# Linear attention and two MLPs on one core: where the second network's weights are split, and the order at the seams

## The reference

```python
# attention, 8 batches x 8 heads x 576 tokens x 64
q_s = exp(q - max(q, axis=-1)); q_s = q_s / (sum(q_s, axis=-1) + 1e-09)
k_s = exp(k - max(k, axis=2));  k_s = k_s / (sum(k_s, axis=2) + 1e-09)
x = q_s @ (k_s^T @ v)                      # -> 4608 tokens x 512
# first network: 512 -> 2048 -> 512
h = x @ w_in
g = np.maximum(h, 0.0) + alpha * np.minimum(h, 0.0)
y = g @ w_out
# second network: 512 -> 1024 -> 512
h = y @ w_in2
solu = h * softmax(h)
ln = (solu - mean(solu)) / np.sqrt(var(solu) + 1e-06) * g_ln
out = ln @ w_out2
```

## Time and profile before

| | us |
|---|---|
| median of 3 runs | 1254.08 (1253.91 to 1256.19) |
| the profiled execution | 1256.36 |
| its span, first to last instruction | 1254.5 |
| TensorE busy | 1221.4 (97%) |
| VectorE busy | 817.5 (65%) |
| ScalarE busy | 507.8 (40%) |
| GpSimd busy | 201.4 (16%) |
| mean granted TensorE clock | 0.988 of full |

### The profile page before, as it was taken

The page is one execution under the profiler, slowest core; times in us unless marked ns, Lnnn a source line. Parts: engine busy times, 40 slices in busy tenths (PEclk is TensorE's granted clock), DMA queues, the critical chain, the costliest instruction groups (busy, mean ns, idle before and its releaser), DMA issues.

```text
span 1254.5 us, 16472 instructions
## 1 busy us (share of the span) xinstructions
PE 1221.4 (97%) x6129; PEld 1010.7 (81%) x6129; DVE 817.5 (65%) x1054; ACT 507.8 (40%) x716; POOL 201.4 (16%) x175
## 2 busy tenths in 40 slices
PE   8889999999999999999999999997999999999998
PEld 7768888888888787888888888985888888888887
DVE  7757577585673556878767697666755655556553
ACT  4433434334343334444344444434543443444432
POOL 5533323133231000000000000011211111111110
PEclk8999999999999999999999999998999999999999
DMA  9686675766744544261452715442544444444432
GB/s 240 210 232 202 176 233 156 222 220 176 227 133 163 204 168 154 104 228 68 152 183 68 228 41 184 153 133 69 176 143 151 144 142 140 150 140 145 143 126 76
DMA packets 199725, 200.74 MB, mean 160 GB/s; under 512 B 62936, under 2 KB 147440, under 8 KB 199536
## 3 DMA queue, kind: packets, MB, share of 16 engines
q1 hardware_dynamic: 199616, 199.91, 50.8%
q10 hardware_dynamic: 48, 0.01, 0.0%
HBM read 116.45 MB, written 83.42 MB: 159 GB/s over the span
## 4 chain that ended last, share of the span: by engine, by line
PE 91%; DVE 4%; DMA 1%; SPq 1%; ACT 1%; issue 1%; POOL 0%; ACTq 0%; DVEq 0%
PE ps_y L1536 10%; PE ps_y L1537 10%; PE ps_y L1538 10%; PE ps_y L1671 5%; PE ps_y L1673 5%; PE ps_y L1672 5%; PE ps_y L1622 5%; PE ps_y L1626 5%; PE ps_y L1624 5%; PE ps_h L1646 3%; PE ps_m L1622 3%; PE ps_h L1647 3%; PE ps_h L1651 3%; PE ps_m L1626 3%; PE ps_m L1624 3%; PE ps_m L1647 2%
## 5 line engine op out<-in xcount | busy, mean ns | idle before, releaser
L1536 PE MATMUL ps_y<-X,W 128*128 128x512 f32 x576 | 228.4, 397 | 3.0 <-DVE gst L1163 3.0
L1537 PE MATMUL ps_y<-X,W 128*128 128x512 f32 x576 | 226.0, 392 | 0.0
L1538 PE MATMUL ps_y<-X,W 128*128 128x512 f32 x576 | 225.9, 392 | 0.0
L1163 DVE SCALAR_TENSOR_TENSOR gst<-gst,nslope,ps_y 128x512 f32<-128x512 f32 x144 | 104.8, 731 | 153.9 <-ACT gst L822 153.8
L822 ACT ACTIVATE gst<-ps_y 128x512 f32<-128x512 f32 x144 | 85.7, 597 | 267.8 <-PE ps_y L1538 250.0
L740 POOL TENSOR_TENSOR x2lb<-x2r,x2hb 128x512 fp32r<-128x512 f32 x36 | 47.1, 1309 | 689.8 <-ACT x2hb L957 689.8
L1536 PEld LDWEIGHTS ps_y<-X,W 128*128 128x128 f32 x576 | 109.1, 189 | 27.1 <-DVE gst L1163 3.4
L1538 PEld LDWEIGHTS ps_y<-X,W 128*128 128x128 f32 x576 | 109.1, 189 | 23.2
L1537 PEld LDWEIGHTS ps_y<-X,W 128*128 128x128 f32 x576 | 109.1, 189 | 22.2
L1622 PE MATMUL ps_y<-rh,WOc 128*128 128x512 f32 (+1 forms) x320 | 117.8, 368 | 1.4 <-DVE rl L1290 1.4
L1624 PE MATMUL ps_y<-rl,WOc 128*128 128x512 f32 (+1 forms) x320 | 117.7, 368 | 0.0
(11 more groups left out here) (176 smaller groups left out, 2303.0 us busy)
## 6 DMA issues: line engine op xcount, KB each, us to landing
g_scratch<-gst SPq DMA_DIRECT2D x144, 256.0 KB, 2.3
RX<-g_scratch SPq DMA_DIRECT2D x36, 512.0 KB, 3.6
z_scratch<-zb SPq DMA_DIRECT2D x35, 512.0 KB, 2.6
zt<-z_scratch SPq DMA_DIRECT2D x140, 128.0 KB, 2.8
RY<-g_scratch SPq DMA_DIRECT2D x18, 512.0 KB, 4.4
RZ<-g_scratch SPq DMA_DIRECT2D x18, 512.0 KB, 5.1
x2r<-y_scratch SPq DMA_DIRECT2D x36, 256.0 KB, 3.1
KK<-k_dram SPq DMA_DIRECT2D x16, 512.0 KB, 6.3
```

Source lines behind the costliest of these rows:

```text
L1163: nc.vector.scalar_tensor_tensor(gst[:, n % 3, :], gst[:, n % 3, :], nslope[:, f:f + 1], ps_y[:, f % 4, :], ALU.mult, ALU.add).then_inc(g_ ...
L1536: nc.tensor.matmul(o, W1[:, f, 0, a, :], x[:, 0, a, :], start=(a == 0), stop=False)
L1537: nc.tensor.matmul(o, W1[:, f, 0, a, :], x[:, 1, a, :], start=False, stop=False)
L1538: mm = nc.tensor.matmul(o, W1[:, f, 1, a, :], x[:, 0, a, :], start=False, stop=(a == KT - 1))
```

## The change

- **Weights of the second network.** `w2_split`, `w2_high`, `w2_low` and their loads are gone. Instead 16 pieces of 128 x 512 (eight of w_in2, eight of w_out2) are loaded into `wst`, split into `whl` (high on ScalarE, low on VectorE) and stored, high and low, to a DRAM scratch `ws_scratch`, three pieces in each of chunks 1 to 5 and one in chunk 6. When the w_out pieces that lie on their place have been used, GpSimd issues six DMAs (two of 2 MB, four of 1 MB) that load `W2` and `WO2`, ready split.
- **Third tile of the second network.** Product 1 of tile 2 goes to the first two banks of `ps_y` (`h_bank`), and waits for `c12_ok` in place of `solu_ok`. For tiles 0 to 3 the orders of ScalarE and VectorE are written out.
- **First chunk.** `k_transpose` from f = 1 to 3, `k_broadcast` 3 to 5, `k_columns` 2 to 3, `k_sub` 4 to 6, third `q_sum` 6 to 7, `k_exp` 7 to 8, `kv_product` and what follows it one step later; the low halves of the first two q tiles for chunk 1 on VectorE instead of GpSimd.
- **Seams.** In chunk 7 the `xrg` split moves from f = 3 to 6 and 7, the w_out pieces from f = 6, 9, 12, 15 to 8, 11, 14 and 1 of chunk 8; in chunk 8 from 5, 9, 13 to 4, 8, 12. The first two units of phase 2 are split ahead of the PReLUs of f = 14 and 15 instead of both ahead of f = 15.

```diff
+        def h_bank(m, r):
+            if isinstance(m, int) and m == 0 and r == 2:
+                return ps_y[:, 0:2, :]
+            return (ps_m, ps_h)[r % 2][:, :, :]
...
+        WS_LOAD, WS_SPLIT = (1, 6, 10), (4, 10, 13)
+        def ws_piece(c, i):
+            n = 3 * (c - 1) + i
+            return n if c > 0 and n < WS else None
...
+            def load_ws(n):
+                if n < 2:
+                    sp.wait_ge(w_lo, NF)
+                else:
+                    sp.wait_ge(ws_lo, n - 1)
...
+                sp.dma_start(wst[:, n % 2, :], src).then_inc(ws_in[n % 2], 16)
+            def store_ws(n):
+                sp.wait_ge(ws_lo, n + 1)
+                sp.dma_start(ws_dram[n].rearrange("s p n -> p s n"), whl[:, :, :].bitcast(F32)).then_inc(ws_st, 16)
...
+                    if f in WS_LOAD and ws_piece(c, WS_LOAD.index(f)) is not None:
+                        load_ws(ws_piece(c, WS_LOAD.index(f)))
+                    if f - 1 in WS_SPLIT and ws_piece(c, WS_SPLIT.index(f - 1)) is not None:
+                        store_ws(ws_piece(c, WS_SPLIT.index(f - 1)))
...
+            pool.wait_ge(ws_st, 16 * WS)
+            for n in range(2):
+                pool.wait_ge(b_used, ends(LAST_U, n))
+                pool.dma_start(W2[:, n, :, :].rearrange("p a (h n) -> p (a h) n", h=2),
+                               ws_dram[0:2 * KT, n, :, :].rearrange("m p n -> p m n")).then_inc(w2_in, 16)
+            half = NF2 // 2
+            for n in range(2):
+                pool.wait_ge(b_used, ends(LAST_U, 2 + n))
+                for i in range(2):
+                    pool.dma_start(WO2[:, n * half:(n + 1) * half, i, :],
+                                   ws_dram[2 * KT + n * half:2 * KT + (n + 1) * half, i, :, :]
+                                   .rearrange("m p n -> p m n")).then_inc(wo2_in, 16)
...
+            def ws_high(n):
+                act.wait_ge(ws_in[n % 2], 16 * (n // 2 + 1))
+                if n > 0:
+                    act.wait_ge(ws_st, 16 * n)
+                if n < 2 * KT:
+                    nc.scalar.activation(whl[:, 0, :], wst[:, n % 2, :], ACT.Copy).then_inc(ws_hi, 1)
...
             for f in range(NF):
-                if f == NF - 1:
-                    for t in UNITS[:EARLY]:
-                        b_high(t)
+                if f >= NF - EARLY:
+                    b_high(UNITS[f - (NF - EARLY)])
                 negative(LAST, f)
-                if f in (5, 9, 13):
-                    wo_high(4 + (5, 9, 13).index(f))
+                if f == 1:
+                    wo_high(3)
+                if f in (4, 8, 12):
+                    wo_high(4 + (4, 8, 12).index(f))
...
                     if t.u == LAST_U:
-                        if t.k in (2, 3):
-                            w2_split(2 * (t.k - 2))
-                            w2_split(2 * (t.k - 2) + 1)
                         if t.k in (4, 5):
...
+            def ws_low(n):
+                dve.wait_ge(ws_hi, n + 1)
+                if n < 2 * KT:
+                    nc.vector.tensor_tensor(whl[:, 1, :], wst[:, n % 2, :], whl[:, 0, :].bitcast(F32),
+                                            ALU.subtract).then_inc(ws_lo, 1)
...
                 if first and r == 0:
-                    pe.wait_ge(w2_lo, KT)
+                    pe.wait_ge(w2_in, 32)
                     pe.wait_ge(c11_ok, PAIRS + 1)
...
+                if first and r == 2:
+                    pe.wait_ge(c12_ok, 2 * (PAIRS + 1))
+                if not (first and r < 3):
                     pe.wait_ge(solu_ok, i - 1)
```

More of the change, by code:

```diff
@@ L74, in linear_attention_two_mlps @@
         X = (X0, X1)
-        (qTh, qTl, kvh, kvl, KK, Q, QN, V, _, kb, qz, wst, kmax, kmt, kvf, qR, xr, arows, kx, ky, kw, kwt, km, ks, kr,
+        (qTh, qTl, kvh, kvl, KK, Q, QN, V, _, kb, qz, wst, whl, kmax, kmt, kvf, qR, xr, arows, kx, ky, kw, kwt, km, ks, kr,
          qm, qs, qe, qr) = place(
@@ L201, in linear_attention_two_mlps @@
         y22_st = sem("y22_st")
-        w2v_in = sem("w2v_in")
-        w2a_in = sem("w2a_in")
-        w2_hi = sem("w2_hi")
-        w2_lo = sem("w2_lo")
+        ws_in = [sem(f"ws_in{i}") for i in range(2)]
+        ws_hi = sem("ws_hi")
+        ws_lo = sem("ws_lo")
+        ws_st = sem("ws_st")
+        w2_in = sem("w2_in")
+        wo2_in = sem("wo2_in")
         x2_in = [sem(f"x2_in{i}") for i in range(4)]
@@ L727, in _ @@
                 w_low(f)
-            for j in range(KT):
+            for j in range(2, KT):
                 q_low(1, j)
@@ L1008, in out_copy, with tiles @@
                 nc.scalar.activation(ost[:, r % 2, :], ps_y[:, 2 + r % 2, :], ACT.Copy).then_inc(o_ok, 1)
-            def tiles(m, first=False, second=False, last=False):
+            def tiles(m, second=False, last=False):
                 for r in range(4):
                     if r >= 2:
-                        zt_high(m, r - 2, first=first)
-                    elif not first:
+                        zt_high(m, r - 2)
+                    else:
                         zt_high(m - 1, r + 2)
@@ L1018, in tiles @@
                         x2_high(m + (r + 2) // 4, (r + 2) % 4)
-                    if first and r < 2:
-                        for f in range(4 * r, 4 * r + 4):
-                            w2_high(f)
                     square_tile(m, r)
                     if r == 3:
-                        out_copy(m, 0, first=first, last=last)
-                    elif not first:
+                        out_copy(m, 0, last=last)
+                    else:
                         out_copy(m - 1, r + 1, first=(second and r == 0))
-            tiles(0, first=True)
+            exp_tile(0, 0)
+            x2_high(0, 2)
+            square_tile(0, 0)
+            exp_tile(0, 1)
+            x2_high(0, 3)
+            square_tile(0, 1)
+            exp_tile(0, 2)
+            x2_high(1, 0)
+            zt_high(0, 0, first=True)
+            square_tile(0, 2)
+            zt_high(0, 1, first=True)
+            exp_tile(0, 3)
+            x2_high(1, 1)
+            square_tile(0, 3)
+            out_copy(0, 0, first=True)
             tiles(1, second=True)
@@ L1228, in _ @@
                         if f == 6:
+                            k_sub(b)
+                        if f == 7:
                             q_sum(b, 2)
@@ L1270, in _ @@
                 prelu(B - 1, f)
-                if f == 3:
-                    for j in range(KT):
+                if f in (6, 7):
+                    for j in range(2 * (f - 6), 2 * (f - 5)):
                         dve.wait_ge(xh_ok, 4 * B + j + 1)
```

182 lines of the change are left out of this document (92 added, 90 removed).

## The result

The changed kernel takes 1251.49 us (median of 10 runs, 1249.44 to 1253.61); the kernel before, run beside it, 1256.26 us (10 runs, 1253.83 to 1258.75). The ratio is 0.9962, with a 95% interval of 0.9952 to 0.9972: faster by 0.38%, 4.8 us. The forecast was 7.9 us less, so the sign was right, and two fifths of the forecast gain are missing. In absolute time 1251.49 us is 5.3 more than the forecast 1246.2: 3.1 us are the missing gain, and 2.2 come from the kernel before, whose median over three runs was 1254.08.

A forecast was written before the change was run, and what follows sets the result against it. The prediction took TensorE's waits, and the half-rate clock after long ones, as the bound (TensorE is 91% of the chain). Terms 0 + 0 + 0 + 1.0 - 0.3 - 8.6 = -7.9 us took 1254.08 to 1246.2 us, range 1240 to 1252.

The forecast's parts named there:

- First chunk: Chunk 0: kmax wait goes, but TensorE waits elsewhere, the x product's wait growing 3.2 to 4.6 us; net 0, bounds -2.5, +2.
- The weights' waits of 2 us near 51 us: First chunk: TensorE, now early, waits some 2 us for the eighth weight tile, which came by DMA only at 51.8 us.
- Splits in chunks 1 to 6: Splitting the second network's weights there costs 0, using 3.0 of 3.5 us of slack; bounds 0 and +5 us.
- the nearest deadline: Chunks 1 to 6: the third tile's x product, 3.5 us of slack between its qTl and its start.
- Chunk 7: The 3.0 us gst wait, from g stores behind 5 MB of loads, stays and the clock falls as before; 0.
- Seam: Start of w_out phase: 1.8 us wait goes, unit 2 waits 3.0 for RY; +1.0 us, or 0.65 gain without low clock.
- Last unit group: 801 to 844 us: one 1.35 us wait goes, but GpSimd's loads slow the RX loads; -0.3 us, bounds -1.4 to +2.
- Rival 2: New loads collide with the last group and z reload: RX units wait 2 us each, reload 2.5 more; 1251 us, 15%.
- Second network: First tiles, first product on W2 to second product: splits leave VectorE, 35.2 becomes 26.6 us with low clock; -8.6 us.
- The sum: Whole kernel: 0 + 0 + 0 + 1.0 - 0.3 - 8.6 = -7.9 us, median 1254.08 to 1246.2 us.

The follow-up runs named there:

- three stores: Changed kernel, but each split piece of the second network's weights is stored three times, to three DRAM places, instead of once; 1253.67 us (one time).
- the old banks: Changed kernel, but the second network's third tile is back in the first tile's two banks and waits for that tile's solu; 1249.60 us (one time).
- VectorE's tile order: Changed kernel, but VectorE takes the second network's first tiles one after the other as before, without splits; ScalarE's order kept; 1254.62 us (one time).
- ScalarE's queue: Changed kernel, but ScalarE issues the six W2 and WO2 loads on its own queue, at the same conditions, instead of GpSimd; 1249.39 us (one time).
- all loads behind RX: Changed kernel, but GpSimd's 8 MB of W2 and WO2 loads wait until the last unit group's two RX loads have landed; 1244.51 us median, 4 runs.

## Why the prediction was right or wrong

**First chunk (forecast 0): right.** Measured -0.8 and +0.4 in two parts. The reason holds too: with the reordering undone, in one execution, the chunk's length stays. The weights' waits of 2 us near 51 us were smaller, 0.3 and 0.5, or up to 1.8 in all in other executions; the wait for `qTl` was 5.4 where I had 4.6.

**Splits in chunks 1 to 6 (0): right**, and safer than I had it: 0.5 of 3.5 us of slack used, where the sum said 3.0. I had added VectorE, the two issues and a 512 KB store ahead of the load as if all lay on one path. With three stores the wait came at the tile that I had named as the nearest deadline.

**Chunk 7 (0): right**, 2.94 us of wait as before; that it stood behind the loads ahead of the g stores is shown by the run that spreads them.

**Seam (+1.0): the sum right, +0.7, and its parts right in kind.** The wait of 1.8 at unit 0 went, a wait of 2.5 with the low clock came at unit 2, where I had 3.0. But I credited the early unit parts, among others, with the first, and did not see that they cause most of the second: the RY loads, which I let start 0.4 us earlier, could have started 1.6 us earlier. The sum also hangs on the clock: in the two executions with this seam in which it stayed at full after unit 2's wait (the old banks, VectorE's tile order), the two parts come to -1.2 and -1.3, where I had -0.65 for that case.

**Last unit group (-0.3): wrong, +4.8. This is the step that failed.** The mechanism was named (the RX loads meet GpSimd's and have no slack), its size was not: I took "512 KB alone 3.5 us, shared in half 1.2 to 1.5 more". Measured is 4.3 us more in the median, 3.3 for the first load and 5.3 for the second. And I counted the delay once: 1.05 us off the 1.35 gained, though by my own figure two loads make 2.4 to 3.0, which would have turned the step to about +1.0 to +1.7.

Half a share supposes that the small transfer gets half of the engines from the moment it is issued. The packets show another course: next to nothing for 2.7 and 4 us, and the second load then gets 28% of the bytes, while two loads of WO2 move beside it. What makes up the 2.7 and 4 us before the first bytes stays open.

A sum that comes near is all bytes outstanding at the issue. An estimate from the rows above: bytes move at 378 GB/s (the mean from 812 to 836 us) from some 2 us after the issue at 809.64; a 512 KB load without company lands in 3.6 us, 1.4 for its bytes at that rate and some 2 beside. When the first RX load is issued, at 820.14, 4.2 MB have been issued and 3.2 moved; 1.0 + 0.5 MB take 4.0 us, with the 2 us 6.0; it lands after 6.9. At the second, at 823.02, the first two WO2 loads have come too: 3.0 MB with its own, 8.0 + 2 = 10.0; it lands after 9.8. For ScalarE's queue the same sum gives 5.7 and 9.7 where 5.0 and 8.9 were measured. It is a sum that fits within 1 us, not a mechanism: the second WO2 load was issued ahead of the second RX load and landed after it (833.1 and 832.9), so the RX load does not wait for all that is ahead, and no run varied the order of issues alone.

Shown is that the loads cause it (41.1 us without them), and that it needs neither GpSimd nor its queue. The Trainium skill (Trainium Kernel Development and Optimization, Key Constraints) says that DMAs issued from SP, ACT and POOL run on the same 16 engines and interleave; the run with ScalarE's queue agrees on the first, with 47.5 us, and the packets of both queues between 827 and 832 us on the second. I took interleaving for an even split, which the sentence does not say.

Two things made the error larger. The second RX load meets the WO2 loads as well, so there are two waits, 3.1 and 2.7 us, not one; and after the second the clock fell to 0.69 of full over 4.8 us. My upper bound for the step, +2, took a loss of 1.7 per load at most. Rival 2 was this mechanism (RX late by 2 us each, the reload 2.5 us slower, 1251), at 15%. Only the RX half of it happened, at twice the price; the reload took 6.9 us, against 7.2 before. That its 1251, and the edge of my range, 1252, lie beside the measured 1251.49 is luck: the two halves do not add up as it says, and 2.2 us of the measured time are the other median of the kernel before. As a change it said -3.3 us, where -4.8 came.

**Second network (-8.6): right in kind, -10.8.** The two waits are 0.4 and 1.9 us (forecast 0.7 and 2.3), the start of the second product 24.5 after the first matmul where the chain gave 24.8. Of the 2.2 us on top 1.8 are the low clock which I counted after the 2.3 us wait and which did not follow the 1.9. The chain counted what mattered; the banks, which I did not price apart, are worth nothing (24.51 us without them).

**The sum** had +4.8 instead of -0.3, and -10.8 instead of -8.6. With the other terms that gives 0.7 + 4.8 - 10.8 and -0.4 for the first two chunks = -5.7; the seam and the rest unrounded make it -5.5 us for the profiled pair without the start-up's scatter. The medians say -4.8, the forecast was -7.9.

## What to carry to other kernels

When bulk loads are moved to a free engine's queue, look for the small load with no slack that they will stand beside, and price it by all bytes outstanding at its issue, which here came within 1 us, not by half a share, and count every such load; a wait on that load's landing ahead of the bulk ones was worth 7 us here, more than the change itself. When an edit moves a step ahead of something, follow that something's stores and what is issued behind them: here one low part ahead of a PReLU delayed the next phase's first loads. Undo each part of a change alone before you credit it: two of this change's parts, the early unit parts and the banks, cost something or gave nothing. And undo a part on every engine that it touches, or the number is, like the 3.7 us of the tile order, a price of neither the old order nor the new one.

## What the runs showed of the hardware

The low clock after a wait of TensorE does not follow from the wait's length alone. At one place, unit 2, length and clock go together: after 2.45 to 2.94 us (six executions) the granted clock was 0.57 to 0.69 over 4 us, after 2.41 and 2.43 us (the old banks, VectorE's tile order) it was 1.00, and these two took 1.7 us less from unit 0 to the last group. Elsewhere they do not: in the last group of the changed kernel 3.14 us was followed by full clock and 2.66 by 0.69; and the 1.9 to 2.0 us ahead of the second product were followed by 1.00 in eight executions (the changed kernel among them) and by 0.57 and 0.66 in two (all loads behind RX, and three stores). I had taken 1.8 us as sure to cost the clock, from the earlier trace rows. What else decides it stays open; a forecast should carry it as a term that may or may not come, 1.6 to 1.8 us each time.
